# Hash-masked attention and two expert layers: the hand-over between them, and who splits three weight tiles

## The reference

```
q_bucket, k_bucket = bits of (q @ proj > 0), (k @ proj > 0) as numbers   # 6 bits
scores = q @ k.T / 8, and -1e9 where the buckets differ
attn   = exp(scores - max); attn /= sum(attn) + 1e-9
x      = attn @ v                     -> (1536 tokens, 512)
```

```
h = x @ w_in1; P = a0 + a1 h + a2 h^2 + a3 h^3; Q = 1 + |b0||h| + |b1|h^2
x = (P / (Q + 1e-6)) @ w_out1
h = x @ w_in2; out = (h - tanh(h)) @ w_out2
```

## Time and profile before

| | us |
|---|---|
| median of 3 runs | 805.32 (804.98 to 806.66) |
| the profiled execution | 804.15 |
| its span | 802.3 |
| PE busy | 774.8 |
| DVE busy | 555.9 |
| ACT busy | 477.4 |
| POOL busy | 121.8 |

### The profile page before, as it was taken

How to read it: one execution, slowest core, us unless ns; L and a number is a source line. 1 busy time by engine, 2 the same in 40 slices (tenths; PEclk the granted TensorE clock), 3 DMA queues, 4 the chain that set the end, 5 groups by cost and what they waited for, 6 DMA issues and landing times.

```text
span 802.3 us, 11858 instructions
## 1 busy us (share of the span) xinstructions
PE 774.8 (97%) x3840; PEld 649.4 (81%) x3840; DVE 555.9 (69%) x898; ACT 477.4 (60%) x924; POOL 121.8 (15%) x106
## 2 busy tenths in 40 slices
PE   4999999999999699999999999999999999999998
PEld 3889889889988588887888888888888888888886
DVE  4879989999996899999888888875442322223222
ACT  3879879888886678777666766755332222222221
POOL 5333533543535300000000000000000000000000
PEclk8899999999999899999999999999999999999999
DMA  5767676677464420000000033230000100001001
GB/s 112 155 166 160 148 176 160 151 174 173 118 169 112 147 103 0 1 2 0 1 1 15 14 91 105 79 105 14 0 1 1 53 1 1 0 1 53 0 1 53
DMA packets 64603, 56.54 MB, mean 70 GB/s; under 512 B 31664, under 2 KB 50352, under 8 KB 64560
## 3 DMA queue, kind: packets, MB, share of 16 engines
q1 hardware_dynamic: 62848, 55.52, 27.1%
q10 hardware_dynamic: 1712, 0.46, 0.3%
HBM read 29.57 MB, written 3.19 MB: 41 GB/s over the span
## 4 chain that ended last, share of the span: by engine, by line
PE 83%; DVE 6%; DMA 4%; issue 3%; SPq 2%; POOL 1%; ACT 1%; DVEq 0%; POOLq 0%; ACTq 0%
PE acc L696 34%; PE h_ps L667 33%; PE slot L227 4%; PE turn_ps L324 4%; PE pv_ps L308 3%; PE pv_ps L310 3%; DMA kA<-k_hot 2%; DVE pt_lo L528 2%; DVE row_min L481 2%; DMA softmax_scale<-row_inv 1%; DVE q_hot L503 1%; PE aux_ps L240 1%; PE aux_ps L249 1%; DVE x_pair L512 1%; DMA q_nat<-in_q 0%
## 5 line engine op out<-in xcount | busy, mean ns | idle before, releaser
L667 PE MATMUL h_ps<-x_hi,win_lo 128*128 128x512 f32 x384 | 151.3, 394 | 1.8 <-DVE win_lo L854 1.8
L667 PE MATMUL h_ps<-x_lo,win_hi 128*128 128x512 f32 x384 | 151.3, 394 | 0.0
L667 PE MATMUL h_ps<-x_hi,win_hi 128*128 128x512 f32 x384 | 151.2, 394 | 0.0
L717 ACT ACTIVATE g_hi<-pol 128x512 fp32r<-128x512 f32 x96 | 60.8, 634 | 131.2 <-PE acc L696 105.1
L846 DVE TENSOR_TENSOR g_lo<-pol,g_hi 128x512 fp32r<-128x512 f32 x96 | 65.9, 686 | 101.1 <-ACT g_hi L717 100.9
L528 DVE TENSOR_TENSOR pt_lo<-turn_ps,pt_hi 128x384 fp32r<-128x384 f32 x192 | 98.0, 551 | 14.8 <-ACT pt_hi L434 13.4
L434 ACT ACTIVATE pt_hi<-turn_ps 128x384 fp32r<-128x384 f32 x192 | 84.1, 490 | 27.1 <-PE turn_ps L324 26.0
L481 DVE TENSOR_REDUCE row_min<-slot 128x1 f32<-128x768 f32 x96 | 90.6, 944 | 7.2 <-PE slot L227 7.2
L410 ACT ACTIVATE E<-slot,row_min 128x768 f32<-128x768 f32 x96 | 87.3, 910 | 2.8 <-DVE row_min L481 2.8
L667 PEld LDWEIGHTS h_ps<-x_hi,win_lo 128*128 128x128 f32 x384 | 72.2, 188 | 19.0 <-DVE win_lo L854 2.2
L667 PEld LDWEIGHTS h_ps<-x_lo,win_hi 128*128 128x128 f32 x384 | 72.2, 188 | 16.9
(11 more groups left out here) (105 smaller groups left out, 1366.5 us busy)
## 6 DMA issues: line engine op xcount, KB each, us to landing
win_raw<-in_moe_w_in SPq DMA_DIRECT2D x32, 256.0 KB, 3.2
wout_raw<-in_moe_w_out SPq DMA_DIRECT2D x32, 256.0 KB, 2.8
q_nat<-in_q SPq DMA_DIRECT2D x16, 192.0 KB, 3.2
v_nat<-in_v SPq DMA_DIRECT2D x8, 384.0 KB, 4.5
scale<-softmax_scale SPq DMA_DIRECT2D x16, 192.0 KB, 3.1
qA<-q_hi SPq DMA_DIRECT2D x15, 192.0 KB, 2.5
qB<-q_hi SPq DMA_DIRECT2D x15, 192.0 KB, 3.0
qB<-q_lo SPq DMA_DIRECT2D x15, 192.0 KB, 3.2
```

The source lines that it names most:

```text
L667: mm = eng.matmul(h_ps[t % 4][:, :], w[:, ws], columns(x, kt, c), start=kt + n == 0, stop=kt == KT - 1 and n == 2)
L717: eng.activation(g_hi[:, t % TEMPS, :], pol[:, t % TEMPS, :], ACT.Copy).then_inc(mlp_sems["g_hi"], 1)
```

## The change

On PE the last three query tiles are written out by hand (`pe_handover`): g1 tile 0 follows the turning of query tile 9 and waits only for the exponentials in `slot` 0; g1 tile 1 follows tile 10; g1 tile 2 follows tile 11 and waits for `slot` 1. The thirds of group 2 go one after g1 tile 0 and two after g1 tile 1. ACT does `act_step(0)` at query tile 9, `act_reads(1)` and `pv_low` of group 2 at tile 10, ahead of the rounding of query tile 11 and the rest of step 1. DVE does `dve_scale` of the second head at query tile 9 (it was at 10), `dve_step(0)` behind it, `dve_x_sum` of group 2 at tile 10, `dve_step(1)` after tile 11, and the last `dve_x_sum` behind that. GpSimd splits three more tiles (in 4, out 2, in 5), ahead of its last `pool_x`; ACT and DVE no longer do, and the counts that PE waits for follow from that. In the splitting functions of ACT and DVE that are left out below, `EARLY_IN` becomes `POOL_IN` and `EARLY_OUT` becomes `POOL_OUT`.

```diff
--- before.py
+++ after.py
@@ -156,6 +156,11 @@
         LATE = [(kind, j + first) for j in range(J) for kind, first in
                 (("in", EARLY_IN), ("out", EARLY_OUT)) if j + first < J]
         FREE_FIRST, FREE_SCORES = 1, 7
+
+        POOL_TILES = ([("in", j) for j in range(EARLY_IN)] + [("out", j) for j in range(EARLY_OUT)]
+                      + LATE[:3])
+        POOL_IN = sum(kind == "in" for kind, _ in POOL_TILES)
+        POOL_OUT = len(POOL_TILES) - POOL_IN
         for kind, j in LATE:
             (w_in_slot if kind == "in" else w_out_slot)[j] = weight_slot(mlp, f"w{kind}{j}")
         y_sb = [sqr[:, 0, :], sqr[:, 1, :], sqr[:, 2, :], mag[:, 2, :]]
@@ -313,17 +318,8 @@
                 mm.then_inc(sems["pv"], 1)
 
         def pe_att(eng, p, first=False, prepare=True, turn=True, last=False):
-            for n in range(TILES):
-                N = p * TILES + n
-                done, count = exp_done(p, n)
-                eng.wait_ge(done, count)
-                for h in range(2):
-                    eng.wait_ge(sems["pt_lo"], BIAS + 2 * N + h - 1)
-                    for c3 in range(T // 2):
-                        kt = h * (T // 2) + c3
-                        mm = eng.transpose(turn_ps[h][:, c3 * P:(c3 + 1) * P],
-                                           E[:, n % RING, kt * P:(kt + 1) * P], ident[:, :])
-                    mm.then_inc(sems["pt"], 1)
+            for n in range(TILES - G * last):
+                pe_tile(eng, p, n)
                 if first and n < 2:
                     pe_turn(eng, 1, n, 0)
                 if first and n == 2:
@@ -342,16 +338,38 @@
                     pe_pv(eng, p, n // G - 1, n % G)
                 elif not first:
                     pe_pv(eng, p - 1, GROUPS - 1, n)
-                if last and n >= TILES - 2:
-                    if n == TILES - 2:
-                        eng.wait_ge(sems["exp0"], BIAS + T * PAIRS)
-                        eng.wait_ge(sems["exp1"], BIAS + T * PAIRS)
-                    pe_g1(eng, n - TILES + 2)
             if last:
-                pe_g1(eng, 2)
-                for i in range(G):
-                    pe_pv(eng, p, GROUPS - 1, i)
-                pe_g1(eng, 3)
+                pe_handover(eng, p)
+
+        def pe_tile(eng, p, n):
+
+            N = p * TILES + n
+            done, count = exp_done(p, n)
+            eng.wait_ge(done, count)
+            for h in range(2):
+                eng.wait_ge(sems["pt_lo"], BIAS + 2 * N + h - 1)
+                for c3 in range(T // 2):
+                    kt = h * (T // 2) + c3
+                    mm = eng.transpose(turn_ps[h][:, c3 * P:(c3 + 1) * P],
+                                       E[:, n % RING, kt * P:(kt + 1) * P], ident[:, :])
+                mm.then_inc(sems["pt"], 1)
+
+        def pe_handover(eng, p):
+
+            pe_tile(eng, p, TILES - 3)
+            eng.wait_ge(sems["exp0"], BIAS + T * PAIRS)
+            pe_g1(eng, 0)
+            pe_pv(eng, p, GROUPS - 2, 0)
+            pe_tile(eng, p, TILES - 2)
+            pe_g1(eng, 1)
+            pe_pv(eng, p, GROUPS - 2, 1)
+            pe_pv(eng, p, GROUPS - 2, 2)
+            pe_tile(eng, p, TILES - 1)
+            eng.wait_ge(sems["exp1"], BIAS + T * PAIRS)
+            pe_g1(eng, 2)
+            for i in range(G):
+                pe_pv(eng, p, GROUPS - 1, i)
+            pe_g1(eng, 3)
 
 
 
@@ -444,12 +462,14 @@
                     act_turned(eng, 1, n, 1)
                 if prepare and HOT_STEPS.get(n - 2 * first, (0, 0))[0] == 1:
                     act_hot_k(eng, p + 1, HOT_STEPS[n - 2 * first][1])
-                if last and n == TILES - 1:
+                if last and n == TILES - 3:
                     act_step(eng, 0)
+                if last and n == TILES - 2:
+                    act_reads(eng, 1)
+                    act_pv_low(eng, p, GROUPS - 2)
             if last:
-                act_pv_low(eng, p, GROUPS - 2)
+                act_step(eng, 1, reads=False)
                 act_pv_low(eng, p, GROUPS - 1)
-                act_step(eng, 1)
 
 
 
@@ -529,8 +549,12 @@
                                       turn_ps[h][:, 0:HALF].rearrange("r (k n) -> r k n", n=P),
                                       pt_hi[dst].bitcast(F32), ALU.subtract
                                       ).then_inc(sems["pt_lo"], 1)
-                if n in (4, 10):
+                if n in (4, 9 if last else 10):
                     dve_scale(eng, p, n // T)
+                if last and n == TILES - 3:
+                    dve_step(eng, 0)
+                if last and n == TILES - 2:
+                    dve_x_sum(eng, p, GROUPS - 2)
                 if first and n == 2:
                     dve_bits(eng, 1)
                 if prepare and HOT_STEPS.get(n - 2 * first, (1, 0))[0] == 0:
@@ -540,8 +564,8 @@
                 if n + AHEAD < TILES or not last:
                     dve_rowmin(eng, p, n + AHEAD)
             if last:
-                for c in range(GROUPS - 2, GROUPS):
-                    dve_x_sum(eng, p, c)
+                dve_step(eng, 1)
+                dve_x_sum(eng, p, GROUPS - 1)
 
 
 
@@ -611,14 +635,12 @@
                     pool_split_v(eng, p + 1, 0)
                 if n == 10 and turn:
                     pool_split_qk(eng, p + 2, 0)
-                if last and n >= 4 and n - 4 < EARLY_IN + EARLY_OUT:
-                    if n - 4 < EARLY_IN:
-                        j = n - 4
-                        pool_early_weights(eng, loads[f"w_in{j}"], w_in_slot[j], n - 4)
+            if last:
+                for i, (kind, j) in enumerate(POOL_TILES):
+                    if kind == "in":
+                        pool_split_weights(eng, loads[f"w_in{j}"], w_in_slot[j], i)
                     else:
-                        j = n - 4 - EARLY_IN
-                        pool_early_weights(eng, loads[f"w_out{j}"], w_out_slot[j], n - 4)
-            if last:
+                        pool_split_weights(eng, loads[f"w_out{j}"], w_out_slot[j], i)
                 pool_x(eng, p)
 
         def columns(t, kt, c):
@@ -630,7 +652,7 @@
             c, j = divmod(rest, J)
             return layer, c, j
 
-        def pool_early_weights(eng, loaded, slot_, n):
+        def pool_split_weights(eng, loaded, slot_, n):
             raw, hi, lo = slot_
             eng.wait_ge(loaded, 16)
             eng.tensor_copy(hi[:, :], raw[:, :]).then_inc(mlp_sems["early_hi"], 1)
@@ -639,18 +661,18 @@
                               ).then_inc(mlp_sems["early_lo"], 1)
 
         def split_in_count(layer, j):
-            return layer * J + j + 1 - EARLY_IN
+            return layer * J + j + 1 - POOL_IN
 
         def split_out_count(layer, j):
-            return layer * J + j + 1 - EARLY_OUT
+            return layer * J + j + 1 - POOL_OUT
 
 
         def pe_g1(eng, t):
             layer, c, j = place(t)
             _, w_hi, w_lo = w_in_slot[j]
             if c == 0:
-                if layer == 0 and j < EARLY_IN:
-                    eng.wait_ge(mlp_sems["early_lo"], j + 1)
+                if layer == 0 and j < POOL_IN:
+                    eng.wait_ge(mlp_sems["early_lo"], POOL_TILES.index(("in", j)) + 1)
                 else:
                     eng.wait_ge(mlp_sems["w_in_lo"], split_in_count(layer, j))
             if layer == 0 and c == 1 and j == 0:
@@ -673,8 +695,8 @@
             _, w_hi, w_lo = w_out_slot[j]
             hi, lo = g_hi[:, t % TEMPS, :], g_lo[:, t % TEMPS, :]
             if c == 0:
-                if layer == 0 and j < EARLY_OUT:
-                    eng.wait_ge(mlp_sems["early_lo"], EARLY_IN + j + 1)
+                if layer == 0 and j < POOL_OUT:
+                    eng.wait_ge(mlp_sems["early_lo"], POOL_TILES.index(("out", j)) + 1)
                 else:
                     eng.wait_ge(mlp_sems["w_out_lo"], split_out_count(layer, j))
             eng.wait_ge(mlp_sems["g_lo"], t + 1)
...
@@ -765,11 +787,12 @@
                 eng.activation(columns(x_hi, i, c), acc[i][:, :], ACT.Copy, scale=-1.0
                                ).then_inc(mlp_sems["x2_hi"], 1)
 
-        def act_step(eng, t):
+        def act_step(eng, t, reads=True):
             L = TILES_LAYER
             x2 = t % J == SKEW - 1 and J <= t < L + J
             if t < L:
-                act_reads(eng, t)
+                if reads:
+                    act_reads(eng, t)
                 if t >= 2:
                     act_g_hi(eng, t - 2)
                 if x2:
...
@@ -1111,10 +1134,10 @@
                 with eng.Fori(1, PAIRS - 2) as p:
                     dve_att(eng, p)
                 dve_att(eng, PAIRS - 2, turn=False)
-                dve_att(eng, PAIRS - 1, prepare=False, turn=False, last=True)
                 eng.wait_ge(loads["coef"], 1)
                 eng.wait_ge(loads["ready"], 2)
-                for t in range(NT + 1):
+                dve_att(eng, PAIRS - 1, prepare=False, turn=False, last=True)
+                for t in range(2, NT + 1):
                     dve_step(eng, t)
```

(4 more changed lines are left out.)

## The result

The changed kernel takes 798.23 us in the median of 7 runs (797.45 to 800.2), the kernel before 804.98 (7 runs, 801.48 to 806.66). The ratio is 0.9926, with a 95% interval of 0.991 to 0.9943: 0.74% faster. 796.9 was predicted, a gain of 8.4 us; the medians are 6.75 us apart, by the interval 4.6 to 7.2. The profiled execution took 797.45 us with a span of 795.6, where 804.15 and 802.3 stood; the spans differ by 6.7. Of these 0.33 us belong to attention ahead of the change: the turning of query tile 9 starts at 247.09 and stood at 247.42. Lines from L667 on have moved by 22 or 23 (L667 is L689, L696 is L718, L801 is L824 and so on). PE is TensorE, DVE is VectorE, ACT is ScalarE and POOL is GpSimd.

The account below looks back on a forecast made before the run. PE, 97% busy, was taken as the bound, losing 9.1 us at the hand-over while waiting for DVE. Step 3's 6.9 plus 1.48 of lead gave 8.4 us: 805.3 - 8.4 = 796.9, own range 796.2 to 798.5, wider 794.6 to 800.6.

Parts of the forecast that it names:

- PE's path: TensorE's hand-over from query tile 9 to g1 tile 5, which would start 10.2 us earlier if PE waits for nobody.
- step 2: DVE's dve_step(2), to begin at 264.3 behind ACT's reads of h tile 2 and take 5.65 us plus pool_x's surplus.
- step 3: DVE's dve_step(3), forecast to begin at 272.05 where it began at 278.95: 6.9 us earlier.
- my middle value: The 2.1 us that the last pool_x was taken to add to DVE's step 2, between 1.44 and 2.6.
- Tile 11: PE's turning of the last query tile, forecast at 256.35 with 0.4 us of slack; a stall there up to 0.3.
- acc tile 10: Taken as the binding acc tile: PE uses up 1.48 us of DVE's lead there, making the gain 8.4 us.
- the wider ranges: The forecast's own range, 796.2 to 798.5 us, and the one reaching to A and B, 794.6 to 800.6.
- A: Rival: PE never waits for DVE because pool_x and DVE miss each other; gain 10.2 us, time 795.1; 13%.
- B: Rival: a larger wait before acc tile 0 drops the clock to 1.2 GHz again; 799.3 to 800.8 us; 14%.
- C: Rival: TensorE held at 1.2 GHz through the hand-over's chopped matmuls, slower than before; 813 us if whole; 4%.
- D: Rival: ACT's new order keeps g(0) late, g_lo(0) stays near 275; time within 1 us of 805.3; 3%.
- R: Experiments' rival: TensorE's line sets the time; DVE costs only the waits at acc tiles 0 and 1. No chance given.

Follow-up runs that it names:

- e3: Kernel before with only TensorE's new hand-over order, ACT and DVE keeping theirs; ratio to the kernel before 1.0006 (0.9995 to 1.0016).
- e4: Changed kernel with two more tiles (out 3 and in 6) split on GpSimd, five late ones in all; ratio to the kernel before 0.9910.
- e7: Changed kernel with the split of a chunk's sums for layer 2 moved to the head of step 19 on ACT and DVE; ratio to the kernel before 0.9895.
- e6: Changed kernel with ACT reading h tile 2 ahead of the last pv_low copy; ratio to the kernel before 0.9922.
- e5: Changed kernel with the last pool_x on 96 of 768 columns, the rest zeros, only to measure a price; ratio to the kernel before 0.9900.
- e1: Changed kernel with the new order only: GpSimd keeps its six tiles, ACT and DVE split the three others again; ratio to the kernel before 0.9925.
- e2: Kernel before with only the three more tiles split on GpSimd, the old order kept; ratio to the kernel before 0.9969.

## Why the prediction was right, and where it was off

**Right, by its steps.** PE's path: g1 tile 0 at once, g1 tile 4 without its 1.81 us, no half-clock acc tile, and acc tile 0 at 267.71 where 267.42 was forecast. ACT and DVE: the last `x_sum` ended at 263.52 (263.4), step 2 began at 264.14 (264.3), step 3 at 272.26 (272.05). `pool_x` cost DVE 1.50 + 0.93 = 2.4 us; 2.1 was taken, 2.6 was the high end and the result of the rule by which GpSimd and VectorE exclude each other. `x_norm` ended at 265.84 and `sqr` 0.54 us later, as in e3 and e4, where 0.56 stood before; so the trace agrees with that rule (the Trainium skill, SBUF — State Buffer, "Who interferes with whom") more closely than with my middle value. These times are from the start of the span, where tile 9 stood 0.33 us earlier than reckoned; counted from tile 9, acc tile 0 was 0.6 us late and step 3 0.5. Tile 11 was turned without a wait; the three further splits ended at 258.45 (258.5).

**The step that failed**, though the time came out near, is the one that names the place where DVE's line last holds PE. The prediction put it at acc tile 10, where DVE had 1.48 us of lead, and added that to the 6.9 us of step 3: "Behind that PE is full to the end." Up to acc tile 10 this is what happened: it came 85.93 - 78.14 = 7.8 us earlier from tile 9, that is 6.36 (step 3) + 1.43. But acc tile 16 waits for the split of chunk 0's sums, late in step 19, and there the kernel before had no lead at all. So the 1.4 us were given back there, as the 1.46 us of waiting show, and the gain of the whole is that of step 3: 31.53 - 25.17 = 6.36 us, and 0.33 from attention. Had acc tile 16 been read, the forecast would have been 6.9 and 798.4. e7 takes the wait away, and acc tile 16 comes 1.56 us earlier.

The size of step 3's advance was a smaller miss: 6.36 us from tile 9 against 6.9. Of that, 0.3 is `pool_x` at 2.4 in place of 2.1 us (it did not stretch four instructions by up to 0.65 each, but two, by 1.50 and 0.93), and 0.2 the start of step 2, 17.05 behind tile 9 where 16.88 was reckoned. The 0.33 us that attention happened to be shorter hid a part of it in the span, and that was luck. So was it that the median of the kernel before came out at 804.98 in place of the 805.32 of the first runs. Even so 798.23 lies above the 796.4 to 797.7 that the prediction's terms gave (its low end, 1.44 in place of 2.1, makes 796.2 when it is worked out), and the 8.4 us lie outside the measured 4.6 to 7.2; only the wider ranges, to 798.5 and 800.6, hold the time.

**The rivals.** A asked for `pool_x` and DVE to miss each other; they meet wherever either is moved (e4, e6). B and C, the lower clock, did not come: the granted clock was 1.00 in each window shown. D did not come either: acc tile 0 started 7.6 us earlier. R is refuted by e7, and by the steadiness of DVE's line over PE's in the table; e5 leans against it, e6 parts nothing. What stays open: how often the 0.1 us race between `sqr` and `x_norm` goes which way from run to run; there is one trace of each kernel, so the shares of a microsecond or less in the table rest on one draw each.

## What to carry to other kernels

When a stage hands over to a saturated one, follow the second engine's line to the last place that waits for it, not to the place where its pace changes; look for the consumer that needs a result late in a step, such as the reuse of an accumulator at a chunk's end. A place with no wait in the trace of before can have no slack either: compare the producer's end with the consumer's start there. And work put on GpSimd is not free beside VectorE: count the VectorE instructions with both inputs in SBUF that it will meet, at up to the whole length of GpSimd's instruction each (`sqr` lost 2.08 us beside an `x_norm` of 2.23 in e3), and cut that instruction or place it where VectorE waits.

## What the runs showed of the hardware

A VectorE instruction with two SBUF inputs that waited for a GpSimd instruction ended 0.54 to 0.56 us behind it, whatever the length of the wait (surplus 0.65, 1.5, 1.6 and 2.08 us); instructions that read PSUM kept 0.68 to 0.75 us. GpSimd waits as well when it is second: `x_norm` took 2.23 to 2.24 us when it was first, 2.77 to 2.85 behind `sqr`. The surplus that one and the same `pool_x` put on VectorE was 1.4 us before, 2.4 in the changed kernel, 3.1 in e1, e4 and e6 and 3.2 in e3, so its place decides nearly as much as its being there at all. PE waits of 1.81, 1.50 and 1.46 us left the granted clock at 1.00 in the stretch behind them (kernel before, e6, changed kernel). Behind 4.56 us (e2) and 4.80 us (before) it was 0.50, the 1.2 GHz level, and behind the 4.37 us ahead of g1 tile 4 in e3 it was 0.62 on average.
